# Moving the first decay clamps from GpSimd to VectorE, and GpSimd's masks and constants ahead of its decay work

## The reference, cut to what matters

```python
def _attn_ref(q, k, v, f_logit):          # B, H, S, D = 4, 8, 768, 48
    f = 1.0 / (1.0 + np.exp(-f_logit))
    state = np.zeros((B, H, D, D))
    for t in range(S):
        state = f[:, :, t, :, None] * state + np.einsum('bhd,bhe->bhde', k[:, :, t], v[:, :, t])
        y[:, :, t] = np.einsum('bhd,bhde->bhe', q[:, :, t], state)
    return y
def reference(...):
    x = _attn_ref(...)                    # then 3072 tokens of 384
    x = _moe_ref(x, ...)                  # 8 experts, 2 of them per token
    return _moe2_ref(x, ...)              # (silu(xn @ w_gate) * (xn @ w_val)) @ w_out
```

## Time and profile before

| | us |
|---|---|
| three runs | 1318.1, 1324.99, 1319.17 |
| their median | 1319.17 |
| the profiled execution, its own time | 1315.64 |
| its span | 1314.0 |
| PE busy | 1246.3 (95% of the span) |
| DVE busy | 859.2 (65%) |
| POOL busy | 454.3 (35%) |

### The profile page before, as it was taken

How to read it: one execution, slowest core, us unless ns; L and a number is a source line. 1 busy time by engine, 2 the same in 40 slices (tenths; PEclk the granted TensorE clock), 3 DMA queues, 4 the chain that set the end, 5 groups by cost and what they waited for, 6 DMA issues and landing times.

```text
span 1314.0 us, 26515 instructions
## 1 busy us (share of the span) xinstructions
PE 1246.3 (95%) x8915; PEld 1148.2 (87%) x8916; DVE 859.2 (65%) x1939; ACT 458.8 (35%) x982; POOL 454.3 (35%) x376
## 2 busy tenths in 40 slices
PE   4899999999899999999999999599999999999998
PEld 3787887877798999989999898499999999999997
DVE  6888898885477878778787787344444544444433
ACT  3565566554222232222322222332332323233221
POOL 8558787654623506060536440310010101010000
PEclk9999999999999999999999999799999999999999
DMA  6233333253613131313313510210010101010000
GB/s 213 66 105 119 125 115 120 82 178 107 228 69 139 41 144 36 144 48 132 144 36 120 184 44 25 78 37 28 28 54 1 55 18 38 18 36 18 0 18 18
DMA packets 36175, 105.46 MB, mean 80 GB/s; under 512 B 4992, under 2 KB 20352, under 8 KB 33664
## 3 DMA queue, kind: packets, MB, share of 16 engines
q1 hardware_dynamic: 27504, 56.41, 13.0%
q0 software_dynamic: 8592, 47.98, 10.3%
HBM read 77.83 MB, written 26.54 MB: 79 GB/s over the span
## 4 chain that ended last, share of the span: by engine, by line
PE 76%; POOL 9%; DVE 7%; ACT 4%; issue 4%; DMA 1%; DVEq 0%; POOLq 0%; ACTq 0%
PE pD L1750 12%; PE pD L1859 10%; PE pA L1859 10%; PE pS L1782 8%; PE pA L1782 8%; PE pA L1873 7%; PE pA L1559 5%; PE pA L1750 4%; PE pS L1873 3%; PE pA L1764 2%; POOL fT L563 1%; PE pX L1724 1%; POOL prods L598 1%; DVE W L1070 1%; POOL we L688 1%
## 5 line engine op out<-in xcount | busy, mean ns | idle before, releaser
L1496 DVE TENSOR_TENSOR gs<-pD,sig 128x384 f32<-128x384 f32 x96 | 53.5, 557 | 199.6 <-ACT sig L1005 199.6
L1246 DVE STREAM_TRANSPOSE pA<-pD 32x128 f32<-32x128 f32 x416 | 138.3, 332 | 54.5 <-PE pD L1750 48.7
L739 POOL DMA_INDIRECT pair<-y_sorted,y_row x48 | 46.5, 969 | 340.7 <-DVE z L1475 271.7
L1246 DVE STREAM_TRANSPOSE pA<-pA 32x128 f32<-32x128 f32 x400 | 133.0, 332 | 44.0 <-PE pA L1750 38.4
L1559 PE MATMUL pA<-W 64*128 64x128 f32 x1920 | 141.6, 289 | 16.3 <-DVE W L1070 12.2
L909 ACT ACTIVATE hidH<-pA 128x512 fp32r<-128x512 f32 x110 | 65.5, 599 | 250.0 <-DVE pA L1246 246.4
L1559 PEld LDWEIGHTS pA<-W 64*128 64x128 f32 x1920 | 119.9, 192 | 34.8 <-DVE W L1070 18.7
L1750 PE MATMUL pD<-we,xsH 128*128 x462 | 146.0, 397 | 2.8 <-issue 2.8
L1782 PE MATMUL pA<-we,hidH 128*128 (+1 forms) x464 | 120.7, 341 | 0.0
L1005 ACT ACTIVATE sig<-pD 128x384 f32<-128x384 f32 x96 | 47.2, 491 | 210.4 <-PE pA L1859 210.4
L1070 DVE TENSOR_TENSOR W<-W,prods 128x512 f32<-128x512 f32 (+1 forms) x120 | 98.8, 829 | 28.9 <-PE pA L1559 26.8
(11 more groups left out here) (260 smaller groups left out, 2887.1 us busy)
## 6 DMA issues: line engine op xcount, KB each, us to landing
stage<-w POOLq DMA_DIRECT2D x14, 1536.0 KB, 8.9
qk<-qk_t SPq DMA_DIRECT2D x24, 512.0 KB, 3.7
xs<-x_sorted SPq DMA_DIRECT2D x55, 192.0 KB, 2.4
y_sorted<-yo SPq DMA_DIRECT2D x55, 192.0 KB, 1.9
fT<-f_t SPq DMA_DIRECT2D x12, 512.0 KB, 4.3
vN<-v_n SPq DMA_DIRECT2D x24, 256.0 KB, 2.7
out<-fin SPq DMA_DIRECT2D x8, 576.0 KB, 2.8
stage<-w SPq DMA_DIRECT2D x2, 1536.0 KB, 9.5
```

The lines of the kernel that those rows point to most:

```text
L739: pool.indirect_dma_start(out=pair[:, j, k], out_offset=None, in_=y_sorted[:, :], in_offset=bass.IndirectOffsetOnAxis(ap=y_row[:, t * TS + ...
L1246: ins = dve.transpose(by_32[1][32 * q:32 * (q + 1), :, i], by_32[0][32 * i:32 * (i + 1), :, q])
L1496: dve.tensor_tensor(gs[:], pD[:, f % 2 * 512:f % 2 * 512 + TT], sig[f % 2][:], ALU.mult).then_inc(s_u, 1)
```

## The change

POOL loses its clamps of pairs 0 and 1. DVE does them instead: the first after three of its clears, the second after all of them, with a semaphore of their own, `s_clamp0`. POOL begins with all its masks and constants, those that stood behind `clamp(1)` included, and only then does `merge_inner(0)`. Its clamp of pair 2, which stood at the head of body 0, now stands behind `products(1)`. ACT waits for `s_clamp0` at pairs 0 and 1 and for `s_clamp` from pair 2 on. The DMAs and PE's program are the same.

```diff
@@ gpsimd
-            clamp(0)
             pool.memset(ident[:], 0.0)
...
             pool.affine_select(out=ident[:], in_=ident[:], pattern=[[-1, P]], compare_op=ALU.not_equal,
                                fill=1.0, base=0, channel_multiplier=1).then_inc(s_const, 1)
-            merge_inner(0)
-            turn_first(0)
-            turn_first(1)
-            products(0)
-            clamp(1)
             pool.affine_select(out=before[:], in_=before[:], pattern=[[1, P]], compare_op=ALU.is_gt,
                                fill=0.0, base=0, channel_multiplier=-1)
...
             pool.iota(region_row[:], pattern=[[0, 2], [REGION, E]], base=0, channel_multiplier=0,
                       allow_small_or_imprecise_dtypes=True).then_inc(s_const, 1)
+            merge_inner(0)
+            turn_first(0)
+            turn_first(1)
+            products(0)
 
             def body(k):
...
-                if is_pair(k + 2):
+                if is_pair(k + 2) and k:
                     clamp(k + 2)
                 if is_pair(k + 1):
                     merge_inner(k + 1)
                     turn_first(2 * k + 2)
                     turn_first(2 * k + 3)
                     products(k + 1)
+                if k == 0:
+                    clamp(2)
@@ scalar
-                act.wait_ge(s_clamp, k + 1)
+                if k < 2:
+                    act.wait_ge(s_clamp0, k + 1)
+                else:
+                    act.wait_ge(s_clamp, k - 1)
+                if k == 1:
+                    act.wait_ge(s_fg, 1)
                 act.activation(fs[:], fT[k % 3][:], ACT.Exp, scale=-1.0).then_inc(s_exp, 1)
@@ vector
-            for t in (*aT, *stateB, hits, zero):
+            def clamp(k):
+
+                dve.wait_ge(s_f[k], 16)
+                dve.tensor_scalar(fT[k][:], fT[k][:], F_MIN, None, ALU.max).then_inc(s_clamp0, 1)
+
+            for t in aT[0:3]:
+                dve.memset(t[:], 0.0)
+            clamp(0)
+            for t in (aT[3], *stateB, hits, zero):
                 dve.memset(t[:], 0.0)
             for t in (ones[:], ones_row[:], more_than[:, :, 0:1]):
                 ins = dve.memset(t, 1.0)
             ins.then_inc(s_clear, 1)
             dve.memset(to_next[:], 0.0).then_inc(s_g2, 1)
+            clamp(1)
             dve.wait_ge(s_const, 2)
```

More of the change, by code:

```diff
@@ L314, in program @@
         s_clamp = sem("s_clamp")
+        s_clamp0 = sem("s_clamp0")
         s_exp = sem("s_exp")
```

## The result

| | before | changed |
|---|---|---|
| median, us | 1320.8 (8 runs, 1316.52 to 1324.99) | 1312.9 (8 runs, 1310.61 to 1314.81) |
| ratio, 95% interval | | 0.995, 0.9936 to 0.9965 |
| profiled execution, its own time and span | 1315.64, 1314.0 | 1313.5, 1311.8 |
| DVE's start of pair 1 (the mark) | 42.67 | 36.25 |

The change makes the kernel 7.9 us faster by this comparison, from 1320.8 to 1312.9; the forecast was 1313.2 from a median of 1319.17. The two profiled executions are only 2.2 us apart at the end, though 6.4 us at the mark.

What follows compares the result with a forecast made beforehand. PE holds 76% of the chain, but POOL's preparation bounds its first stretch; gains of 3.35, 0.55, 0.7 and 1.4 us sum to 6.0, taking the 1319.17 us median to 1313.2, range 1308.8 to 1318.0.

Steps and rivals of the forecast that it cites:

- Part 1: Start of merge_inner(0): DVE's 0.87 us clamp and earlier masks move it from 13.39 to 10.03, gaining 3.35 us.
- Part 2: Clamp of pair 1 on DVE: ends by 10.7 us at the latest, before turn_others(0) can start; costs nothing.
- Part 3: POOL without a gap between the two pairs' products: merge_inner(1) at 19.2 us, DVE's wait gone, gain 0.55 us.
- Part 4: DVE beside POOL's products: 2.5 us of slowdown removed, 1.8 added over levels 1 to 3, net gain 0.7 us.
- low stretch: PE's granted clock at 0.52 from 36.6 to 40.0 us before the change, taken as costing 1.4 us.
- the prediction's own sign: Crowding estimate counts as wrong if doublings between 20 and 30 us are unslowed or their steps grow over 2.3 us.
- Part 5: PE's half-clock stretch before pair 1 taken as gone or moved where mostly hidden: gain 1.4 us, bounds 0 and 1.4.
- The sum: DVE's start of pair 1 comes 6.0 us earlier, from 3.35, 0.55, 0.7 and 1.4, and the end likewise.
- POOL's configuration: Rival, 14 in 100: masks start late after POOL's configuration, losing some or all of the early start; 1316 us.
- the crowding costs what the gap gave: Rival, 20 in 100: low clock only moves, levels beside POOL's products pay 2.3 us or more; 1315.7 us.
- The later stages: Rival, 4 in 100: stages after the first swallow the lead, no change, 1319 us.
- PE did not stay at 1.2 GHz: Negates a rival, 3 in 100: PE stays at half clock through pair 0 into pair 1, slower, 1327 us.

Runs made afterwards that it cites:

- changed_again: The changed kernel run once more with no edit; 1311.03 us against 1315.61 before, ratio 0.9966.
- before_again: The kernel before the change, run and profiled once more with no edit; 1315.92 us in one run.
- pool_order_only: The kernel before with only POOL's new order, all clamps staying on POOL; 1314.98 us, ratio 0.9996.
- hold_pair1: The changed kernel with POOL waiting ahead of merge_inner(1) for DVE's level 2 doubling of tile 1; 1312.18 us, ratio 0.9972.
- clamp1_on_pool: The changed kernel with the clamp of pair 1 back on POOL, behind products(0); 1312.48 us, ratio 0.997.
- clamps_only_breaks: dve_clamps_only plus waits of POOL for its own last result inside pair 1's run; 1310.53 us, ratio 0.9959.
- halves: The changed kernel with pair 0's load, clamp, ACT steps and merge by tiles, DVE's pair 1 clamp behind turn_others(0); 1312.24 us, ratio 0.9966.
- halves_breaks: halves plus POOL waits for its own results between the parts of pair 0; 1313.0 us, ratio 0.9961.
- no_clamp2: The changed kernel with POOL's clamp of pair 2 left out, so some work is missing; 1314.2 us in one run.
- dve_clamps_only: The kernel before with the clamps of pairs 0 and 1 on DVE, POOL's order nearly as before; 1314.47 us, ratio 0.999.
- clamps_only_shift: dve_clamps_only plus three POOL waits behind products(0) that only move its run by 0.14 us; 1315.06 us in one run.

## Why the prediction was right

- **Part 1, the start of `merge_inner(0)`: as worked out.** 10.10 against 10.03. The clamp was 1.06 us instead of 0.87; alone it is 0.69 (both rows of DVE above). That is what the estimate from the Trainium skill's figure (VectorE: DVE Perf Modes, The perf-mode tier table) had. Beside POOL's masks either side can pay: in changed_again the clamp took 0.69 us and the mask at 4.62 took 1.02 instead of 0.63. The decays landed 0.12 us earlier and made up for most of the longer clamp. The gain was 3.29 us.
- **Part 2: cost nothing, as said.** The second clamp ends at 9.84, and `turn_others(0)` waits for POOL until 11.78.
- **Part 3: as said.** `merge_inner(1)` at 19.27 against 19.2, with no idle time. The two clamps behind the products, covered by 5 us in the forecast, are done at 33.53, and ACT wants the first at 38.28.
- **Part 4: about the right size, for another reason.** The forecast put 1.8 us of slower doublings beside POOL's products. There it was 4 x 0.07 = 0.3 us. Two doublings of 1.49 and 1.52 us at the starts of POOL's clamps added 2 x 0.8 = 1.6: together 1.9. One such doubling was already there before (26.20, 1.37 us), so the net added cost is nearer 1.2. (The second, at 40.35, came only with the low stretch.) By the prediction's own sign, doublings between 20 and 30 us free of the slow-down, this part was nearly wrong. The removed part was right: `turn_others` of pair 1 fell from 1.138 to 0.680.
- **Part 5, the clock: the step with the weakest argument.** That 1.4 was forecast and 1.55 measured is in part luck: 0.96 is DVE's wait for PE, 0.53 the doubling at a clamp's start that nobody had in the sum. The forecast also took the low stretch as a part of the program, and before_again has none. Whether the change removes it stays open, but the profiles lean that way. Five kernels' profiles have pair 1's products begin at 25.8 us or later (before, before_again, pool_order_only, hold_pair1, clamp1_on_pool), and three of them show half the clock for 3.4 us ahead of the mark. Six have them begin by 22.8 us and no hold behind them (both of the changed kernel, clamps_only_breaks, halves, halves_breaks, no_clamp2), and none does. (dve_clamps_only and clamps_only_shift have one too, behind PE's idle time in the hold.)
- **The sum: 6.0 forecast, 6.42 seen at the mark**, the same mark in both. Set against the run of before without the low stretch and counted from the first clamp's start, the changed kernel gains 36.26 - 31.51 = 4.75 us, and 5.2 by changed_again. The parts as measured give the same without the clock: 3.29 less the 0.12 us of earlier decays, 0.55, and 2.5 - 1.2 = 1.3, together 5.0. The two comparisons of whole times, 7.9 and 4.6 us, lie to both sides. That the measured 1312.9 is 0.3 us from the forecast is therefore luck too: the base was 1.6 us higher than the one it was counted from, and the gain larger.
- **A slip in the range.** The forecast's upper end is given as 7.3 and as 7.5 us; with no cost of crowding part 4 makes it 6.0 + 1.8 = 7.8. Nothing hangs on it.
- **The rivals.** POOL's configuration was not late: the first mask stands at 1.98, right behind the memsets, and the 6 us that the Trainium skill has for a first call (GPSIMD Engine Reference, Instruction dispatch) show for none of these instructions. That the crowding costs what the gap gave is out for this order, though dve_clamps_only shows that it can, by one hold. The prediction had no such hold among its rivals; that none fell into the changed kernel was not foreseen. The later stages swallowed nothing that changed_again didn't keep. PE did not stay at 1.2 GHz.

## What to carry to other kernels

When an engine's preparation, and not its input, sets the start of the chain, give the first steps to an engine that idles, and expect the gain at a mark near the start to be about the gain in the medians; two single profiles of one kernel can still differ at the end by as much (the changed kernel's two by 4.3 us). One profiled execution can hold a low clock stretch of over a microsecond on the chain that the next doesn't: take a second profile before putting a price on it, and a comparison with an interval where the gain is under one per cent. Where GpSimd and VectorE work side by side, look for VectorE instructions many times their usual length, and try a wait of GpSimd for its own result in its longest run without a pause.

## What was unexpected

**Holds.** A VectorE instruction with two inputs can be kept out through a whole run of GpSimd instructions: 5.40 us (dve_clamps_only), 5.22 (clamps_only_shift), 4.53 (halves) and 3.59 (pool_order_only), where 0.69 is the usual. In all four it ended 0.54 to 0.55 us behind the start of GpSimd's first pause, however short (0.07 to 0.08 us), and so did the doubling of clamps_only_breaks that a pause let in. In other runs the same kind of meeting goes by turns: 1.14 us on VectorE (hold_pair1), about 1 us instead of 0.63 on GpSimd (clamps_only_breaks). The Trainium skill (SBUF — State Buffer, SBUF: two separate sides) has the two engines share a port pair under an exclusive lock that whoever starts first keeps for its whole instruction. The taking by turns agrees with that, 0.69 against 1.14. The holds through seven instructions go beyond it. What decides between the two is open: VectorE started 0.07 us behind a GpSimd instruction in two of the holds (pool_order_only, halves), but 0.07 and 0.08 us behind one where it was not held (before, the changed kernel), and no rule came out of that.

**Where a clamp costs.** A GpSimd tensor-scalar of 2.8 us slows only the VectorE doubling at its start (1.26 to 1.52 us instead of 0.68), and in the changed kernel and no_clamp2 the ones beside the rest of it not at all. GpSimd can be the one that pays as well: in clamps_only_breaks, where `to_block_ends` had begun 0.11 us ahead of it, the clamp took 3.73 us.
